# Opening of an FFT-mix-FFN kernel: padded x tiles, one tile of batch 1 ahead of the first step, and products of zeros on TensorE

## The chip, the core and the metric

The kernel runs on one NeuronCore of a Trainium2 chip. The metric is the device time in microseconds (us) from launch to end, the median of several executions. Engines are named as in the profile: PE (TensorE matmul), PEld (its weight load), DVE (VectorE), ACT (ScalarE), POOL (GpSimd), SP (SyncE, which here only issues DMAs). SPq and ACTq are DMA issues of SP and ACT.

## The reference

`x` is 2 batches of 3008 tokens by 256 values, all float32.

```python
X = np.fft.rfft(x, axis=1)
Yr = Xr @ w_r - Xi @ w_i + b_r          # Xr, Xi: parts of X
Yi = Xr @ w_i + Xi @ w_r + b_i
Yr, Yi = soft-threshold of each by 0.01
x = np.fft.irfft(Yr + 1j * Yi, n=3008, axis=1).reshape(6016, 256)
h = x @ w_in                            # 256 -> 2048, first layer
x = (np.maximum(h, 0) + alpha * np.minimum(h, 0)) @ w_out
h = x @ w_in2                           # second layer
y = (0 below -1, h above 1, (h + 1)**2 / 4 between) @ w_out2
```

## The kernel before

3008 = 47 * 64, so the transform over tokens is done in two stages. Stage A is a transform of length 47: `x` is laid out by the host as 16 tiles (`TILES`), 8 of each batch (`TILES_PER_BATCH`), each of 94 rows padded to 96 (`ROWS_PAD`) by 1024 columns. `real47(t, banks)` (L1058) multiplies one tile by the 96x96 constant `fwd_sb` in two products of 512 columns (two matmul records each). ACT copies the left half out of PSUM and DVE the right half, both called `copy_a`; ACT's `store_a` (L570) then stores the tile (384 KB) to the DRAM tensor `slots_scratch`. For tile 7, the last of batch 0, the left half is stored from ACT (L574) and the right half from SP (L355).

Stage B goes in 48 steps, two to a pair, 24 steps to a batch. A pair reads `zt` (256 KB, values of all 8 tiles of its batch, from `slots_scratch`) and `gc` (256 KB, constants of its two steps). Per step PE runs `forward` (2 products), `mix` of the step before (12 products with the split weights `wm_hi`, `wm_lo`) and `inverse` of the step before that (one product). ACT and DVE split and threshold between them, and `take_v` copies the result out for its store. So the first step of batch 0 needs all 8 tiles of batch 0 stored, but none of batch 1; the first step of batch 1 (step 24) needs tiles 8 to 15.

`FIRST_TILES` = 11: tiles 0 to 10 go through stage A ahead of step 0. Tiles 11 to 15 are `LATE_TILES`: each goes between `forward` and `mix` of step 1, 4, 7, 10 or 13. SP issues the loads in an order written out by hand (L342 to L365): the left half of x tile 0, `fwd_sb`, its right half, x tiles 1 to 8, `wm_raw` (512 KB), `gc` of pair 0, x tile 9, the bias; then it waits for the products of tile 6 and issues x tile 10; then it waits for the right half of tile 7 and stores it; then it waits until all nine stores of batch 0 have landed (L357) and issues `zt` of pair 0, x tile 11, `zt` and `gc` of pairs 1 and 2, x tile 12. From pair 3 on (loop at L367) each turn issues `zt` (when the forward products that read the slot before are done) and `gc`, in turns 4, 5 and 7 also the late x tile of `LATE_LOADS`, and then waits for a pair of `take_v` before it stores that pair.

`wm_hi` is made by ACT after tile 8 (L584 to L586), `wm_lo` by DVE after tile 9 (L816 to L819); PE waits for `wm_lo` in step 0 (L1208).

After step 47 come the two layers, in blocks of products with split operands (L1123), which the change doesn't touch. Their PSUM banks and SBUF areas are shared with stages A and B; `x_sb` and `a_sb` lie where the weights and token tiles of the layers stand later.

## Time and profile before

| | us |
|---|---|
| median of 3 runs | 1200.5 |
| lowest, highest | 1198.73, 1201.2 |
| the profiled execution | 1200.99 |
| its span, first to last instruction | 1198.9 |
| PE busy in the span | 1174.6 (98%) |
| DVE, ACT, POOL busy | 883.2, 850.3, 682.9 |

Stage A and the wait for step 0 take the first 32 us, the steps until about 170 us, and the two layers the rest. All that the change touches lies ahead of step 14, some 75 us from the start. "Granted clock" is the share of TensorE's full clock that the chip gave it: 1.00 is 2.4 GHz and 0.50 is 1.2 GHz.

### The profile page before, as it was taken

The page shows a single profiled execution, that of the slowest core. Times are in us where ns is not written, and L with a number is a line of the kernel's source. Part 1 is how long each engine was busy: PE and PEld are TensorE (multiplying, and loading weights), DVE is VectorE, ACT ScalarE, POOL GpSimd, SP SyncE. Part 2 cuts the span into 40 slices and gives each one's busy share as a digit, 9 for nine tenths or more (in the row PEclk, how much of TensorE's full clock was granted, in tenths as well). Part 3 has the DMA queues.
Part 4 walks back from the last instruction along what each step waited for, and adds up shares of the span by engine and source line. Part 5 has one row for each costly group of instructions (what it writes and reads, how often), then busy time and mean ns, then how long its engine had stood idle before and what let it go on. Part 6 is the DMA issues. An engine that isn't in the chain of part 4 may idle for free.

```text
span 1198.9 us, 21022 instructions
## 1 busy us (share of the span) xinstructions
PE 1174.6 (98%) x6944; PEld 1135.9 (95%) x6944; DVE 883.2 (74%) x1681; ACT 850.3 (71%) x1874; POOL 682.9 (57%) x714
## 2 busy tenths in 40 slices
PE   7899999999999999999999999999999999999997
PEld 2699889999999999999999999999999999999997
DVE  2577777777777777777778777877778787878765
ACT  2235556767776777767677788888878787878775
POOL 0005635666675757757556656565657565757553
PEclk9899999999999999999999999999999999999999
DMA  9777720211102111112004510101010101000001
GB/s 307 213 223 242 226 71 2 84 43 60 41 27 84 49 54 41 53 58 75 18 2 157 181 51 1 27 1 27 1 27 1 27 1 22 7 17 11 12 16 27
DMA packets 63772, 77.46 MB, mean 65 GB/s; under 512 B 30960, under 2 KB 43376, under 8 KB 63664
## 3 DMA queue, kind: packets, MB, share of 16 engines
q1 hardware_dynamic: 60180, 69.65, 19.3%
q10 hardware_dynamic: 3484, 6.48, 1.6%
q8 instruction: 55, 0.90, 0.3%
q14 instruction: 53, 0.43, 0.1%
HBM read 45.83 MB, written 30.28 MB: 63 GB/s over the span
## 4 chain that ended last, share of the span: by engine, by line
PE 93%; POOL 3%; DMA 1%; ACT 1%; DVE 1%; issue 1%; POOLq 0%; SPq 0%; DVEq 0%; ACTq 0%
PE bank L1123 79%; PE bank L1090 6%; PE bank L1109 2%; PE bank L1066 2%; PE bank L1100 2%; PE bank L1077 2%; POOL g_lo L498 2%; DMA slots_scratch<-a_sb 1%; DMA x_sb<-x 0%; POOL prep_raw L524 0%; POOL xc_lo L473 0%; ACT g_hi L745 0%; DMA fwd_sb<-fwd 0%; ACT prep_hi L768 0%; DVE y_sum L837 0%
## 5 line engine op out<-in xcount | busy, mean ns | idle before, releaser
L498 POOL TENSOR_TENSOR g_lo<-g_sb,g_hi 128x376 fp32r<-128x376 f32 x510 | 505.2, 1001 | 374.0 <-ACT g_hi L745 373.6
L1123 PE MATMUL bank<-g_hi,w_out_hi 128*128 128x376 f32 x1024 | 344.9, 337 | 0.9 <-POOL g_lo L498 0.4
L1123 PE MATMUL bank<-g_lo,w_out_hi 128*128 128x376 f32 x1024 | 342.0, 334 | 0.0
L1123 PE MATMUL bank<-g_hi,w_out_lo 128*128 128x376 f32 x1024 | 341.8, 334 | 0.0
L1123 PE MATMUL bank<-xc_hi,w_in_hi 128*128 128x376 f32 x896 | 302.3, 337 | 0.6 <-DVE partial L902 0.2
L1123 PE MATMUL bank<-xc_hi,w_in_lo 128*128 128x376 f32 x896 | 300.3, 335 | 0.0
L1123 PE MATMUL bank<-xc_lo,w_in_hi 128*128 128x376 f32 x896 | 298.5, 333 | 0.0
L745 ACT ACTIVATE g_hi<-g_sb 128x376 fp32r<-128x376 f32 x512 | 261.0, 510 | 44.2 <-DVE g_sb L939 28.5
L1123 PEld LDWEIGHTS bank<-g_hi,w_out_hi 128*128 128x128 f32 x1024 | 192.4, 188 | 8.8 <-POOL g_lo L498 7.6
L1123 PEld LDWEIGHTS bank<-g_lo,w_out_hi 128*128 128x128 f32 x1024 | 192.3, 188 | 0.0
L1123 PEld LDWEIGHTS bank<-g_hi,w_out_lo 128*128 128x128 f32 x1024 | 192.3, 188 | 0.0
L1123 PEld LDWEIGHTS bank<-xc_hi,w_in_hi 128*128 128x128 f32 x896 | 168.3, 188 | 1.6 <-DVE partial L902 0.5
L1123 PEld LDWEIGHTS bank<-xc_hi,w_in_lo 128*128 128x128 f32 x896 | 168.3, 188 | 0.1
L1123 PEld LDWEIGHTS bank<-xc_lo,w_in_hi 128*128 128x128 f32 x896 | 168.3, 188 | 0.0
L734 ACT ACTIVATE act_a<-bank,half 128x376 f32<-128x376 f32 x192 | 108.8, 566 | 45.6 <-PE bank L1123 44.7
L736 ACT ACTIVATE act_a<-act_a 128x376 f32<-128x376 f32 x256 | 132.9, 519 | 8.1
L939 DVE SCALAR_TENSOR_TENSOR g_sb<-bank,neg_alpha,g_sb 128x376 f32<-128x376 f32 x192 | 115.7, 602 | 2.5 <-ACT bank L730 2.3
L729 ACT ACTIVATE g_sb<-bank 128x376 f32<-128x376 f32 x192 | 91.8, 478 | 35.1 <-PE bank L1123 33.9
L912 DVE TENSOR_TENSOR partial<-u,bank 128x376 f32<-128x376 f32 x128 | 69.4, 542 | 62.8 <-PE bank L1123 61.9
L943 DVE SCALAR_TENSOR_TENSOR g_sb<-bank,act_a 128x376 f32<-128x376 f32 x192 | 104.4, 544 | 5.3 <-ACT act_a L736 1.2
L919 DVE TENSOR_TENSOR h<-partial,bank 128x376 f32<-128x376 f32 x128 | 69.7, 545 | 46.5 <-PE bank L1123 46.4
L730 ACT ACTIVATE bank<-bank 128x376 f32<-128x376 f32 x192 | 92.1, 480 | 0.0
(77 smaller groups left out, 1525.9 us busy)
## 6 DMA issues: line engine op xcount, KB each, us to landing
gc<-group_consts SPq DMA_DIRECT2D x24, 256.0 KB, 4.3
zt<-slots_scratch SPq DMA_DIRECT2D x24, 256.0 KB, 4.2
inverse_scratch<-v_sb SPq DMA_DIRECT2D x24, 256.0 KB, 2.5
ut<-inverse_scratch SPq DMA_DIRECT2D x16, 384.0 KB, 5.1
x_sb<-x SPq DMA_DIRECT2D x15, 384.0 KB, 8.1
slots_scratch<-a_sb ACTq DMA_DIRECT2D x15, 384.0 KB, 6.2
prep_raw<-wpack SPq DMA_DIRECT2D x16, 256.0 KB, 2.6
out<-yt SPq DMA_DIRECT2D x120, 32.0 KB, 1.6
```

Source lines behind the costliest of these rows:

```text
L498: pool.tensor_tensor(g_lo[kind][:, :], g_sb[n % 3][:, :], g_hi[kind][:, :].bitcast(f32), ALU.subtract)\
L729: act.activation(gg, h, ACT.Relu)
L730: act.activation(h, h, ACT.Relu, scale=-1.0).then_inc(act_done, 1)
L734: act.activation(a, h, ACT.Relu, bias=half[:, 0:1], scale=0.5).then_inc(root_ready, 1)
L736: act.activation(a, a, ACT.Square).then_inc(act_done, 1)
L745: act.activation(g_hi[kind][:, :], g_sb[n % 3][:, :], ACT.Copy).then_inc(hi_ready, 1)
L912: dve.tensor_tensor(partial[:, :], u2[:, :], c21_bank[:, 0:N], ALU.add).then_inc(u3_ready, 1)
L919: dve.tensor_tensor(h22[:, :], partial[:, :], c12_bank[:, 0:N], ALU.add).then_inc(h_ready[C22], 1)
L939: dve.scalar_tensor_tensor(out=gg, in0=h_of(kind), scalar=neg_alpha[:, f:f + 1], in1=gg, op0=ALU.mult, op1=ALU.add).then_inc(g_ready, 1)
L943: dve.scalar_tensor_tensor(out=gg, in0=h_of(kind), scalar=1.0, in1=a, op0=ALU.max, op1=ALU.min).then_inc(g_ready, 1)
L1090: last = pe.matmul(y_bank[:, 0:D], xs[s % SLOTS][:, c, at:at + P], ws[:, (part * DC + c) * D:(part * DC + c + 1) * D], start=n == 0, stop= ...
L1123: done = pe.matmul(out_ap, w, g, start=first and n == 0, stop=last_one and n == 2, skip_group_check=unchecked)
```

## The change

- The host pads each x tile to 128 rows (512 KB instead of 384 KB), `x_sb` gets 128 partitions and `fwd_sb` 128 rows with zeros below row 96. Each tile but the first is one transfer as before. The products now contract over 128 rows. `a_sb` and the stores stay at 96 rows.
- `FIRST_TILES` is 9: only tile 8 of batch 1 goes ahead of step 0. Tiles 9 to 15 go into steps 1, 3, 5, 7, 9, 11 and 13. SP loads x tile 9 after `zt` of pair 0, x tile 10 where x tile 12 stood, and x tiles 11 to 15 in turns 3 to 7 of its loop.
- SP stores the right half of tile 7 ahead of `gc` of pair 0 and `wm_raw`, which stood ahead of it, and the bias goes behind x tile 9. The wait for the products of tile 6 is gone.
- `wm_hi` and `wm_lo` are made after the copies of all nine first tiles, and PE waits for `wm_lo` ahead of the first `mix` instead of in step 0.
- PE runs 2 products of zeros (96x96 by 96x512, `WARM_PRODUCTS`) before it waits for `fwd_sb`, and 3 more (`WAIT_PRODUCTS`) after tile 8, ahead of step 0. They write `xt_bank[0]`, which step 0 overwrites. DVE clears the operand first, ahead of its other clears.

```diff
-FIRST_TILES = TILES_PER_BATCH + 3
-LATE_TILES = {1: FIRST_TILES, 4: FIRST_TILES + 1, 7: FIRST_TILES + 2, 10: FIRST_TILES + 3, 13: FIRST_TILES + 4}
-LATE_LOADS = {4: FIRST_TILES + 2, 5: FIRST_TILES + 3, 7: FIRST_TILES + 4}
+FIRST_TILES = TILES_PER_BATCH + 1
+LATE_TILES = {1 + 2 * n: FIRST_TILES + n for n in range(TILES - FIRST_TILES)}
+LATE_LOADS = {3 + n: FIRST_TILES + 2 + n for n in range(TILES - FIRST_TILES - 2)}
+WARM_PRODUCTS = 2
+WAIT_PRODUCTS = 3
...
-        x_sb = sb("x_sb", [ROWS_PAD, TILES, TILE_COLS], scope=step_a)
+        x_sb = sb("x_sb", [P, TILES, TILE_COLS], scope=step_a)
...
-        fwd_sb = sb("fwd_sb", [ROWS_PAD, ROWS_PAD], scope=fft)
+        fwd_sb = sb("fwd_sb", [P, ROWS_PAD], scope=fft)
...
-            for t in range(1, TILES_PER_BATCH + 1):
+            for t in range(1, FIRST_TILES):
                 load_x(t)
-            sp.dma_start(wm_raw[:, :], wmix).then_inc(wm_in, 16)
-            load_matrices(0)
-            load_x(TILES_PER_BATCH + 1)
-            sp.dma_start(bias_sb[:, :], bias).then_inc(bias_in, 16)
-            sp.wait_ge(a_done, 2 * (TILES_PER_BATCH - 1))
-            load_x(TILES_PER_BATCH + 2)
             t = TILES_PER_BATCH - 1
             sp.wait_ge(a_right, t + 1)
             sp.dma_start(az_rows[0, 0:ROWS_PAD, t * TILE_COLS + HALF_COLS:(t + 1) * TILE_COLS],
                          a_tile(t)[:, HALF_COLS:]).then_inc(a_stored[0], 16)
+            load_matrices(0)
+            sp.dma_start(wm_raw[:, :], wmix).then_inc(wm_in, 16)
             sp.wait_ge(a_stored[0], 16 * (TILES_PER_BATCH + 1))
             load_values(0)
             load_x(FIRST_TILES)
+            sp.dma_start(bias_sb[:, :], bias).then_inc(bias_in, 16)
...
-                if t == TILES_PER_BATCH:
-                    act.wait_ge(wm_in, 16)
-                    act.activation(wm_hi[:, :], wm_raw[:, :], ACT.Copy).then_inc(wm_hi_ready, 1)
+            act.wait_ge(wm_in, 16)
+            act.activation(wm_hi[:, :], wm_raw[:, :], ACT.Copy).then_inc(wm_hi_ready, 1)
...
+            dve.memset(a_tile(TILES - 1)[:, 0:HALF_COLS], 0.0).then_inc(idle_ready, 1)
             dve.memset(half[:, :], 0.5).then_inc(half_ready, 1)
...
-                if t == TILES_PER_BATCH + 1:
-                    dve.wait_ge(wm_hi_ready, 1)
-                    dve.tensor_tensor(wm_lo[:, :], wm_raw[:, :], wm_hi[:, :].bitcast(f32), ALU.subtract)\
-                       .then_inc(wm_lo_ready, 1)
+            dve.wait_ge(wm_hi_ready, 1)
+            dve.tensor_tensor(wm_lo[:, :], wm_raw[:, :], wm_hi[:, :].bitcast(f32), ALU.subtract)\
+               .then_inc(wm_lo_ready, 1)
...
+            def idle_products(count):
+
+                zeros = a_tile(TILES - 1)
+                for _ in range(count):
+                    pe.matmul(xt_bank[0][0:ROWS_PAD, :], zeros[:, 0:ROWS_PAD], zeros[:, 0:HALF_COLS],
+                              start=True, stop=True)
+
+            pe.wait_ge(idle_ready, 1)
+            idle_products(WARM_PRODUCTS)
             pe.wait_ge(fwd_in, 16)
...
             def mix(s):
+                if s == 0:
+                    pe.wait_ge(wm_lo_ready, 1)
                 pe.wait_ge(xt_lo_ready, s + 1)
...
                 real47(t, [a_bank[(2 * t + part) % 4] for part in range(2)])
+            idle_products(WAIT_PRODUCTS)
             for s in range(STEPS):
                 forward(s)
                 if s in LATE_TILES:
                     real47(LATE_TILES[s], a_bank[0:2])
-                if s == 0:
-                    pe.wait_ge(wm_lo_ready, 1)
-                else:
+                if s:
                     mix(s - 1)
...
-    tiles = np.zeros((TILES, ROWS_PAD, TILE_COLS), x.dtype)
+    tiles = np.zeros((TILES, P, TILE_COLS), x.dtype)
```

## Rows read from the trace of the kernel before

**Rows 1.** The page, parts 1 and 2: busy time, and the clock in 40 slices.
```profile
PE 1174.6 (98%) x6944; PEld 1135.9 (95%) x6944; DVE 883.2 (74%) x1681; ACT 850.3 (71%) x1874; POOL 682.9 (57%) x714
...
PEclk9899999999999999999999999999999999999999
```

**Rows 2.** The chain that ended last, first 60 us: start us, us, what.
```profile
3.32 17.22 PE bank L1066 x32
...
21.27 7.56 DMA slots_scratch<-a_sb
...
28.85 0.39 SPq L322
...
29.28 5.66 DMA x_sb<-x
...
46.47 1.72 PE bank L1066 x4
48.19 1.42 PE bank L1090 x12
49.61 0.43 PE bank L1100 x2
50.05 0.44 PE bank L1077 x4
```

**Rows 3.** PE in order of time: start us, us, line, records [idle before, releaser].
```profile
24.92 1.96 PE L1066 MATMUL bank<-x_sb,fwd_sb 96*96 96x512 f32 x4 [2.69 <-DMA x_sb<-x]
27.65 1.96 PE L1066 MATMUL bank<-x_sb,fwd_sb 96*96 96x512 f32 x4 [0.77 <-DVE a_sb L812]
32.23 1.16 PE L1077 MATMUL bank<-gc,zt 128*128 128x128 f32 x8 [2.63 <-DMA zt<-slots_scratch]
34.98 3.73 PE L1066 MATMUL bank<-x_sb,fwd_sb 96*96 96x512 f32 x4 [1.59 <-DMA x_sb<-x]
```

**Rows 4.** Weight loads of two records and a copy, in order of time.
```profile
9.40 0.28 PEld L1066 LDWEIGHTS bank<-x_sb,fwd_sb 96*96 96x96 f32 x1 [0.57 <-issue]
...
10.49 0.16 PEld L1066 LDWEIGHTS bank<-x_sb,fwd_sb 96*96 96x96 f32 x1 [0.27 <-issue]
...
22.27 0.69 DVE L812 COPY a_sb<-bank 96x512 f32<-96x512 f32 x1 [1.03 <-PE bank L1066]
```

**Rows 5.** Stretches: us, busy PE, PEld, DVE, ACT, POOL, clock, DMA share, GB/s.
```profile
8.00:11.00 3.00, 3.00 (x6) 0.97 (x5) 0.69 (x1) 0.59 (x1) 0.00 (x0) 1.00 1.01 244
14.00:17.00 3.00, 3.00 (x9) 1.14 (x8) 1.06 (x2) 1.05 (x2) 0.00 (x0) 1.00 1.03 416
...
50.00:80.00 30.00, 30.00 (x210) 26.32 (x209) 22.65 (x59) 12.06 (x36) 0.00 (x0) 1.00 0.70 214
...
34.00:35.00 1.00, 0.02 (x1) 0.02 (x1) 0.72 (x3) 0.00 (x0) 0.00 (x0) 0.50 0.95 349
...
40.00:41.00 1.00, 1.00 (x8) 1.00 (x8) 0.00 (x0) 0.00 (x0) 0.00 (x0) 0.71 1.06 265
```

**Rows 6.** The tile wm_raw: ns min/median/max, first and last start us; its load's landing.
```profile
L347 SPq DMA_DIRECT2D wm_raw<-wmix x1: 671/671/671, 6.2 to 6.2; - x1
L586 ACT ACTIVATE wm_hi<-wm_raw x1: 1056/1056/1056, 23.4 to 23.4; 128x1024 fp32r<-128x1024 f32 x1
L818 DVE TENSOR_TENSOR wm_lo<-wm_raw,wm_hi x1: 1211/1211/1211, 27.5 to 27.5; 128x1024 fp32r<-128x1024 f32 x1
...
DMA to landing us min/median/max: 14.8/14.8/14.8
```

**Rows 7.** A store issue of ACT, in order of time.
```profile
30.41 0.31 ACTq L578 DMA_DIRECT2D slots_scratch<-a_sb  x1
```

**Rows 8.** DMA issues from 45 to 80 us: count, KB each, median us to landing.
```profile
inverse_scratch<-v_sb SPq DMA_DIRECT2D x6, 256.0 KB, 2.5
...
slots_scratch<-a_sb ACTq DMA_DIRECT2D x4, 384.0 KB, 3.6
x_sb<-x SPq DMA_DIRECT2D x3, 384.0 KB, 5.0
```

More of the change, by code:

```diff
@@ L206, in fft_mix_ffn_kernel @@
         rims_ready = sem("rims_ready")
+        idle_ready = sem("idle_ready")
         wm_hi_ready = sem("wm_hi_ready")
@@ L1267 @@
     fwd47, inv, group_consts = transform_constants()
+    fwd = np.zeros((P, ROWS_PAD), fwd47.dtype)
+    fwd[:ROWS_PAD] = fwd47
     rows_bias = np.concatenate([np.broadcast_to(v, (N2, D)) for v in (b_r, b_i)], axis=0)
@@ L1274 @@
         "wpack": np.stack(layers),
-        "fwd47": fwd47,
+        "fwd47": fwd,
         "inv47": inv,
```

## The prediction

> **What bounds the kernel now.** I read the page first: PE is busy 98% of the span, and the clock row shows less than full speed only in the second slice, 30 to 60 us [rows 1]. So time can be won only where PE stands still or runs at half clock, and every piece of PE work that is added outside such a place costs its full length. The chain of waits says where the first 60 us go [rows 2]: tiles 0 to 7 on PE from 3.32 to 20.54; the store of the last half tile, issued at 21.27, takes 7.56 us and lands at 28.83; then zt of pair 0 and x tile 11, the latter issued at 29.28 and landed at 34.94. From 34.98 on the chain is PE alone. PE in order of time [rows 3] shows the same from its side: tiles 9 and 10 fall into the wait for the store and cost nothing; PE idles 2.63 us before the two forward products at 32.23 and 1.59 us before tile 11 at 34.98. That tile takes 3.73 us [rows 3], the one at 46.47 takes 1.72 [rows 2].
>
> The clock: the granted clock is 0.50 (1.2 GHz) at 34 us, after PE had been busy for only 1.16 of the 5.4 us from 29.6 to 34.98, and back at 1.00 during 40 to 41 us [rows 3, 5], 5.4 us after tile 11 began. At the start the profile's clock column shows 1.00, but the weight loads of the tiles take 0.28 us with 0.57 idle ahead of them, 0.85 us a record, at 9.40, and 0.16 with 0.27, 0.43 us a record, at 10.49 [rows 4]: PE there runs at half speed until about 9.8, 6.5 us after its first product. A product is two records, 1.7 us at half clock and 0.86 at full.
>
> DMA: from 8 to 11 us only x loads move, at 244 GB/s with all 16 engines busy; from 14 to 17 loads and stores together move 416 GB/s [rows 5]. wm_raw was issued at 6.2 and landed 14.8 us later [rows 6], so SP's queue was full of loads when the last store was put behind them.
>
> **The change part by part.** The sum is made against the profiled execution, 1200.99 us, of which the span is 1198.9; it lies 0.5 us above the median of the runs shown, and I take the difference as carried over.
>
> 1. Warm products. The clear of 96x512 on DVE isn't in the trace; the copy of the same shape from PSUM is 0.69 us [rows 4], so it is between 0 and 0.7, and PE starts at about 1.3. Two products at half clock take 2 x 1.72 = 3.4 us, to 4.75. The first real product, which started at 3.32, starts at 4.75: a loss of 1.4. The clock then comes up 5.4 to 6.5 us after 1.3, at 6.7 to 7.9, instead of at 9.8. Tiles 0 to 7 hold 16 products of 0.86 us at full clock, 13.8 us, plus half of the time spent at half clock: 4.75 + 13.8 + (7.3 - 4.75)/2 = 19.8, against 20.54 now (20.4 by the same formula). Gain 0.7; bounds: a gain of 1.0 with the clock up at 6.7, and a loss of 1.4 if it comes up only 6.5 us after the first real product, as now.
>
> 2. Padding. At 244 GB/s a tile of 384 KB (0.393 MB) takes 1.6 us. What 512 KB in 128 rows takes alone isn't in the trace. From below: at the 416 GB/s that the engines reach in the later stretch, 1.26 us. From above: at 244 GB/s, 2.15 us. I take about 1.5, since the engines show that they can move 416 while the 96-row loads alone get 244; what holds those is then not the engines but the spread of the rows. Then x tile 8 is in by 16 us, PE never waits for a tile, and padding is worth nothing in itself. In the words of the Trainium skill (SBUF — State Buffer, Door 1: The DMA port swizzle), rows 0 to 63 reach only half of the SBUF's ports and rows 64 to 127 the other half; a 96-row tile would then be limited by the 64 rows on the first half and cost as much as one of 128. The low rate of the 96-row loads agrees; that 128 rows are better no row here shows.
>
> 3. The last store. SP's issues ahead of it drop from 16 to 11: wm_raw, gc, the bias and x tiles 9 and 10, 1.7 MB, no longer stand before it, against 1.2 MB of padding. The queues hold the stores alone once the x loads are in. Nine x tiles are 4.7 MB; at 1.5 us each they end near 16. About 1.2 MB of stores wait by then, PE makes 223 GB/s of them (0.393 MB in 1.72 us), and the engines move up to 416, so little is left at 20.5. The half tile is issued at 20.6 and lands between 22.9 (2.3, just under the 2.5 of 256 KB stores [rows 8]) and 24.2 (3.6, a 384 KB store there). I take 23.3, against 28.83 [rows 2]: gain 5.5.
>
> 4. zt of pair 0. Issued at 28.85 it landed at 32.2, 3.4 us later [rows 2, 3], with next to nothing queued in front. Now gc and wm_raw (0.79 MB), issued right after the store, are partly ahead of it, and the store of tile 8 beside it: 0.3 to 0.6 us more. It lands at 27.0; bounds 26.2 and 28. Two forward products follow as now.
>
> 5. x tile 9, issued behind zt. Tile 11 landed 2.7 us after zt, with a store of 384 KB (tile 10's) beside it [rows 7]. Now no store is beside it, but 512 KB are to move: 1.5 to 2.7, I take 2.0. PE starts the late tile of step 1 at 29.0 instead of 34.98: 6.0 earlier.
>
> 6. wm_lo. wm_raw lands at about 25.5; ACT's split and DVE's take 1.06 and 1.21 us [rows 6], so wm_lo is there by 28, ahead of the first mix at 30.7 at the earliest. ACT's wait for wm_raw holds back its first split_xt, which isn't due before 27.6; DVE's wait for wm_hi holds back nothing else. Nothing, as long as wm_raw is not a further 2.7 us late.
>
> 7. Two more late tiles. Tiles 9 and 10 leave a wait in which they were free and enter steps in which PE is busy all of the time (30.00 of 30 us from 50 to 80 [rows 5]). Each adds 1.72 us [rows 2]: a loss of 3.44, with no doubt about it. A step without a tile is 1.43 + 0.43 + 0.44 = 2.30 us.
>
> 8. Wait products. Three at full clock are 2.6 us, from the end of tile 8 (21.5) to 24.1, ahead of zt's landing: they cost nothing unless zt comes before 24.1. What they are worth is the clock at 29. Without them PE would idle from 21.5 to 27; with them it idles 24.1 to 27.0, works 1.16, idles about 0.9. That is 1.16 us of work in 4.9, hardly more than the 1.16 in 5.4 that let the clock fall now, and less than the 1.96 us in 5.4 from 22.2 to 27.65 that did not [rows 3]. So I take it that the clock falls again, and 5.4 us at half clock, 2.7 us lost, stay as they are. Bounds: 0 and a gain of 2.7.
>
> 9. Late loads. zt, gc, a pair's store, a tile's store and x (512 KB) are 1.70 MB in two steps of 6.33 us, 269 GB/s, where 50 to 80 us now show 214 at a share of 0.70: a share of up to 0.88 by bytes. An x tile is issued some 1.9 us after the end of a step with a tile and is needed 9.1 us after that end, so it has 7.2 us; the loads now take 5.0 [rows 8]. It fits; nothing. A load above 7.2 us would not (rival D).
>
> Sum: 6.0 - 3.44 = 2.5 us gained, and items 1, 3 and 4 are in the 6.0. All later work is behind PE and moves up with it. 1200.5 - 2.5 = 1198.0.
>
> **The rivals.** A, the forecast: the clock falls again, 1198.0, own range 1196.8 to 1199.3 by items 3 to 5. Chance 0.42.
>
> B: the clock stays up over the shorter gap, since zt comes by 26.5 or since a gap of 2.7 us, like the one at 24.92, leaves it [rows 3]. Then 2.7 more is won, less about 0.5: tile 9 starts at 29.0, step 3 needs x tile 10 at 34.9, and some 1.9 MB are in front of it. 1200.5 - 2.5 - 2.2 = 1195.8; with zt 1 us earlier 1194.8. In its favour: PE's work before the gap ends later relative to zt than now. Against: the gap and the work in it look like those at 30 to 35. The Trainium skill (TensorE: Matmul & The Clock Gate, Why this matters for your kernels) says that the clock only drops after a sufficiently long gap between bursts, which would make this the outcome; the drop at 34 us came over two gaps of 2.63 and 1.59 with work between. Chance 0.30.
>
> C: padding costs its bytes, 2.15 us a tile at 244 GB/s. Loads alone until 13 us, then half of 416 beside stores: x tile 7 lands near 20.5, PE ends it at 22.3, the store lands at 25.3, zt at 28.9, x tile 9 at 31.1. That is 3.9 earlier than now, less 3.44: 0.5 gained, 1200.0. For it: rate is all that the row gives. Against: 416 GB/s on the same engines. Chance 0.12.
>
> D, the other side: x tiles 12 to 15 come late to their steps. The place is the wait in real47 of steps 7, 9, 11, 13; it decides once a load takes over 7.2 us instead of 5.0, which a DMA share near 1 would bring: 269 GB/s stand against 214/0.70 = 306 by [rows 5], and 128 rows need only cost somewhat more than their bytes. Each then costs 1 to 1.8 us; at 1.4, 5.6 us in all, 1198.0 + 5.6 = 1203.6. It passes no change at 0.6 us a tile and 0.2% slower at 1.25. Chance 0.10.
>
> E: the products of zeros don't bring the clock up sooner, 2.1 us worse in item 1, of which the time that the stores get to drain hides about 1: 1199.1. Chance 0.06.
>
> **How the numbers follow.** A difference of 0.2%, 2.4 us, is about what a measurement of this kernel can tell from none, so faster is below 1198.1 and slower above 1202.9. A lies at this edge: 0.42 x 0.55 = 0.23 to faster, 0.19 to the same; B 0.29 faster, 0.01 the same; C 0.11 the same, 0.01 slower; E 0.01 faster, 0.05 the same; D 0.02 the same, 0.08 slower. Faster 0.53, same 0.38, slower 0.09. The range goes from 1194.2 (B with an early zt) to 1201.0 (C with its bounds), which leaves out D and the ends.
>
> **What would show it.** Step 1: weight loads 0.43 us apart from about 7.5 us on. Step 2: over 300 GB/s between 4 and 11 us; 244 would be rival C. Step 3: the landing of SP's last store at about 23.3. Steps 4 and 5: forward products at 27.0, tile 9 at 29.0. Step 7: seven tiles at 1.72 us in the chain. Step 8: a granted clock of 0.50 somewhere between 27 and 34; 1.00 throughout is rival B. Step 9: no wait of PE for x_sb after 30 us; some in steps 7 to 13 are rival D. The prediction is wrong if the first mix is not 5 to 7 us earlier than now, or if later steps take longer than 2.30 and 4.02 us.

## The result, and the profile after

| | before | after |
|---|---|---|
| median, both kernels in turn on one chip | 1200.7 | 1202.8 |
| lowest, highest of 22 runs each | 1198.39, 1203.02 | 1200.64, 1207.63 |
| ratio, 95% interval | | 1.002 [1.0011, 1.0028] |
| the profiled execution, its span | 1200.99, 1198.9 | 1201.93, 1199.9 |

The change makes the kernel 2.1 us slower. The forecast was 2.5 us faster, and 1202.8 lies above the range.

The page of the changed kernel: the span, the busy time of each engine, and the clock row.

```profile
span 1199.9 us, 21044 instructions
PE 1179.9 (98%) x6954; PEld 1139.0 (95%) x6954; DVE 883.8 (74%) x1682; ACT 850.4 (71%) x1874; POOL 682.8 (57%) x714
...
PEclk9999999999999999999999999999999999999999
```

PE is busy 5.3 us longer than before. The five products of zeros alone are 6.4 us (3.7 for the first two, 2.7 for the last three, below); most of that lies in waits, but the first two put off the first real product, from 3.32 us [rows 2] to 4.96. The half-clock mark has left the second slice [rows 1], but that isn't all gain: the next views tell.

PE in order of time, the changed kernel (columns as in rows 3).

```profile
1.45 3.73 PE L1058 MATMUL bank<-a_sb 96*96 96x512 f32 x4 [1.45 <-DVE a_sb L803]
4.96 2.96 PE L1074 MATMUL bank<-x_sb,fwd_sb 128*96 128x512 f32 x4
8.18 10.54 PE L1074 MATMUL bank<-x_sb,fwd_sb 128*96 128x512 f32 x24 [0.26 <-DMA x_sb<-x]
18.88 1.96 PE L1074 MATMUL bank<-x_sb,fwd_sb 128*96 128x512 f32 x4 [0.16 <-DMA x_sb<-x]
21.25 1.96 PE L1074 MATMUL bank<-x_sb,fwd_sb 128*96 128x512 f32 x4 [0.41 <-DMA x_sb<-x]
23.04 2.74 PE L1058 MATMUL bank<-a_sb 96*96 96x512 f32 x6
29.38 2.08 PE L1085 MATMUL bank<-gc,zt 128*128 128x128 f32 x8 [3.60 <-DMA zt<-slots_scratch]
31.25 3.46 PE L1074 MATMUL bank<-x_sb,fwd_sb 128*96 128x512 f32 x4
```

The two warm products (1.45 to 4.96), nine tiles, the three wait products (to 25.8), then 3.60 us of nothing until `zt`, the forward products at 29.38 and tile 9 at 31.25. Before, the same points were 32.23 and 34.98 [rows 3]. Tile 9 thus starts 3.7 us earlier, where 6.0 were forecast.

SP's issues of the same stretch, and those that store pairs 2 and 7 of batch 0 (here and below "the third store" and "the eighth store").

```profile
21.59 0.34 SPq L352 DMA_DIRECT2D slots_scratch<-a_sb  x1
21.98 0.42 SPq L319 DMA_DIRECT2D gc<-group_consts  x1
22.45 0.48 SPq L355 DMA_DIRECT2D wm_raw<-wmix  x1
24.82 0.38 SPq L325 DMA_DIRECT2D zt<-slots_scratch  x1
25.24 1.21 SPq L314 DMA_DIRECT2D x_sb<-x  x1
...
55.97 0.38 SPq L329 DMA_DIRECT2D inverse_scratch<-v_sb  x1
...
84.18 0.38 SPq L329 DMA_DIRECT2D inverse_scratch<-v_sb  x1
```

The same two stores in the profile of before:

```profile
59.13 0.37 SPq L326 DMA_DIRECT2D inverse_scratch<-v_sb  x1
...
85.62 0.38 SPq L326 DMA_DIRECT2D inverse_scratch<-v_sb  x1
```

When the eighth store is issued all late tiles of either kernel are done, so its time is a ruler for everything that the change touches. The change was 3.16 us ahead at the third store, and 1.44 ahead at the eighth, with one late tile more in between (1.72). What is left of the span after the eighth store is 1113.3 us in the kernel before (1198.9 - 85.6) and 1115.7 in the changed one (1199.9 - 84.2), though nothing there was edited. So two questions: why is the lead at 85 us only 1.4, and where do 2.4 us go behind it?

### The profile page after: what moved, and what is told of

Same layout as the page of the kernel before. It is cut to its first block, busy times and chain, and to the rows that moved or that the text cites. A ratio compares the mean times of both kernels' runs of the same rounds, so it can differ in the third digit from the quotient of the medians.

```text
span 1199.9 us, 21044 instructions
## 1 busy us (share of the span) xinstructions
PE 1179.9 (98%) x6954; PEld 1139.0 (95%) x6954; DVE 883.8 (74%) x1682; ACT 850.4 (71%) x1874; POOL 682.8 (57%) x714
## 4 chain that ended last, share of the span: by engine, by line
PE 78%; POOL 3%; issue 1%; ACT 0%; DVE 0%; POOLq 0%; DVEq 0%; ACTq 0%
PE bank L1133 76%; PE bank L1119 2%; POOL g_lo L498 2%; POOL prep_raw L524 0%; POOL xc_lo L473 0%; POOL prep_raw L509 0%; ACT g_hi L744 0%; ACT prep_hi L767 0%; POOL prep_raw L514 0%; POOL prep_raw L512 0%; POOL prep_raw L510 0%; POOLq L138 0%; ACT bank L729 0%; DVE yt L965 0%; ACT act_a L733 0%
```

## Experiments

Times are medians; "before" is the kernel before, run in turn with the variant on the same chip. The experiments were run in four sets on three chips, and each set has its own "before"; across sets the ratios are the safer comparison. The interval of a ratio is 0.0008 to 0.0018 to either side, 1 to 2 us, so two variants are told apart only from some 2 us on; smaller differences rest on the profiles, and each of those is one execution. No kernel here leaves out a part of the computation: products of zeros and of `wm_raw` go to banks that are overwritten.

**The parts one by one.** No products of zeros:

```diff
-WARM_PRODUCTS = 2
-WAIT_PRODUCTS = 3
+WARM_PRODUCTS = 0
+WAIT_PRODUCTS = 0
```

> The changed kernel without products of zeros (0 instead of 2 and 3). The changed kernel's median is 2.1 us above before (ratio 1.002), though in its profile the steps run 1.44 us ahead of before up to step 34. Theory 1, the zeros pay: the half-clock stretch at the start lasts some 1.4 us longer for real products and the one ahead of step 0 comes back, so 1 to 3 us slower than the changed kernel, ratio to before 1.003 to 1.0045. Theory 2, the zeros cost (they push back the first product and bring nothing): ratio 1.000 to 1.001.

Measured 1203.79, before 1200.82: 1.002 [1.0007, 1.0033]. The last half tile was stored at 23.57 instead of 21.59, tile 9 began at 33.45 instead of 31.25, the eighth store went out at 86.76 instead of 84.18. In time 1.0 us is left of that by medians and nothing by ratios (1.002 for both), inside the noise: neither expectation is confirmed.

Unpadded, the rest of the change as it is (`fwd_sb` is back to 96 rows too):

```diff
-        x_sb = sb("x_sb", [P, TILES, TILE_COLS], scope=step_a)
+        x_sb = sb("x_sb", [ROWS_PAD, TILES, TILE_COLS], scope=step_a)
...
-    tiles = np.zeros((TILES, P, TILE_COLS), x.dtype)
+    tiles = np.zeros((TILES, ROWS_PAD, TILE_COLS), x.dtype)
```

> The changed kernel with x tiles of 96 rows as before; all else as changed. Theory 1, padding is neutral or helps (378 GB/s in the stretch 8 to 11 us of the changed kernel against 244 before): ratio to before 1.002 to 1.003. Theory 2, the padded bytes are what costs (x loads beside the stores, late tiles): ratio 1.000 or below, and the last store lands before 24.0 instead of 24.8.

Measured 1202.23, before 1200.82: 1.001 [0.9992, 1.0027]. SP's store and its `zt` in this kernel:

```profile
20.25 0.32 SPq L352 DMA_DIRECT2D slots_scratch<-a_sb  x1
...
23.58 0.38 SPq L325 DMA_DIRECT2D zt<-slots_scratch  x1
```

Both are issued 1.3 us earlier than with 128 rows (21.59, 24.82). Most of that lead is gone at tile 9 (30.99 against 31.25), since `zt` took 5.5 us here, and the time is the same within the noise.

The reverse, the kernel before with padding alone:

> The kernel before with x tiles padded to 128 rows and nothing else. Theory 1: TensorE sets the pace of tiles 0 to 7 anyway, so the ratio is 0.9995 to 1.0005. Theory 2, the added bytes stand ahead of the last store: it lands later than 28.83 by 1 to 3 us, ratio 1.001 to 1.0025.

Measured 1201.73, before 1200.82: 1.0004 [0.999, 1.0019]. Its weight loads show the price, first this kernel and then the kernel before:

```profile
8.73 0.39 PEld L1066 LDWEIGHTS bank<-x_sb,fwd_sb 128*96 128x96 f32 x2 [2.79 <-DMA x_sb<-x]
```

```profile
5.99 0.28 PEld L1066 LDWEIGHTS bank<-x_sb,fwd_sb 96*96 96x96 f32 x1 [0.57 <-DMA x_sb<-x]
```

x tile 1 is used at 8.73 instead of 5.99, PE stands, and the last half tile is stored at 23.58 instead of 21.27. In this profile padding is not neutral in stage A. The wait for the store doesn't hide it: the store landed at 31.4 instead of 28.8 and `zt` at 34.4 instead of 32.2, as the second expectation had it. But the clock was back earlier after tile 11, the eighth store went out only 0.7 us later (86.33), and in time nothing is told apart.

**Is it the long wait?** A real tile in place of two products of zeros, x tile 9 loaded right behind the store, and `wm_raw` behind `zt`:

```diff
-FIRST_TILES = TILES_PER_BATCH + 1
+FIRST_TILES = TILES_PER_BATCH + 2
-WAIT_PRODUCTS = 3
+WAIT_PRODUCTS = 1
...
+            load_x(TILES_PER_BATCH + 1)
             load_matrices(0)
-            sp.dma_start(wm_raw[:, :], wmix).then_inc(wm_in, 16)
             sp.wait_ge(a_stored[0], 16 * (TILES_PER_BATCH + 1))
             load_values(0)
+            sp.dma_start(wm_raw[:, :], wmix).then_inc(wm_in, 16)
```

> The changed kernel, but tile 9 (the second of batch 1) goes ahead of step 0 too, with one product of zeros behind it instead of three; its x load stands right behind the last store and wm_raw behind zt of pair 0. Six late tiles instead of seven. Theory 1, each late tile costs 1.72 us of TensorE and the wait for zt has room for it: 1.7 us below the changed kernel or more, ratio to before 1.000 to 1.001. Theory 2, what costs is not the late tiles: ratio 1.002 as the changed kernel. A zt that lands over 1.7 us later because of the x load ahead of it would also give 1.002.

Measured 1201.27, before 1200.82: 1.0004 [0.999, 1.0018]. Eighth store at 84.00, against 84.18 in the change. The real tile found no free time: its load landed at 28.1, PE stood 5.2 us for it and ran it at half clock, and `zt`, which had landed at 30.4, was first read at 33.2. By its interval the time is told apart neither from before nor from the change.

**The late tiles alone.** The kernel before with 9 first tiles and seven late ones, every load where it was (`wm_lo` is made after the copy of tile 8, the last of the first tiles, instead of tile 9):

```diff
-FIRST_TILES = TILES_PER_BATCH + 3
-LATE_TILES = {1: FIRST_TILES, 4: FIRST_TILES + 1, 7: FIRST_TILES + 2, 10: FIRST_TILES + 3, 13: FIRST_TILES + 4}
+FIRST_TILES = TILES_PER_BATCH + 1
+LATE_TILES = {1 + 2 * n: FIRST_TILES + n for n in range(TILES - FIRST_TILES)}
...
```

> The kernel before with the late tiles of the change alone: tiles 9 and 10 go into steps 1 and 3, the others into 5 to 13, their loads and all other DMAs stay where they are, no padding, no zeros. Theory 1, a late tile costs its 1.72 us of TensorE and its place ahead of step 0 was free: 3.4 us slower than before, ratio 1.0025 to 1.003; more if the longer idle stretch ahead of step 0 keeps the clock down longer. Theory 2, the steps hide part of it: ratio below 1.0015.

Measured 1203.44, before 1201.4: 1.0015 [1.0002, 1.0029]. It costs about as much as the whole change. `zt` landed at 30.0, against 32.2 in the profile of before: with two tiles fewer the queues are emptier.

**A clock fall outside the change.** At about 148 us the first token products wait 2.43 us for DVE in both kernels. Granted clock and busy times of PE from 140 to 160 us (columns as in rows 5), before and then after:

```profile
140.00:160.00 20.00, 16.71 (x131) 15.90 (x130) 14.34 (x38) 10.46 (x30) 11.54 (x13) 1.00 0.30 93
```

```profile
140.00:160.00 20.00, 16.72 (x118) 15.86 (x117) 12.88 (x34) 9.07 (x26) 10.47 (x11) 0.91 0.30 93
```

In the changed kernel the clock fell there, in the one before it did not. To take this away from both, five products are put into step 42, in the stretch ahead of the wait:

```diff
+                if s == 42:
+                    for _ in range(5):
+                        pe.matmul(xt_bank[(s + 1) % SLOTS][:, 0:D], wm_raw[:, 0:P], wm_raw[:, 0:D],
+                                  start=True, stop=True)
```

On the kernel before:

> The kernel before with five products (128x128 by 128x256, read from wm_raw, into a PSUM bank that is free then) in step 42, in the 2.43 us in which TensorE waits near 148 us for DVE. All up to 145 us is as before, so its profile is a second look at the front of the kernel before. Theory 1: the clock falls at that gap in some executions (it did in the profile of the changed kernel, 140 to 160 us at 0.91, 1.5 us lost, and not in that of before), so the fill gives 0.3 to 1.5 us, ratio 0.999 to 0.9997. Theory 2: the fall has nothing to do with the gap, ratio 1.000 or, if the fill ends after the wait, 1.0003. For the front: if the profile shown of before was a typical execution, tile 11 starts at 35.0 and the third pair's store at 59.1; if it was a slow one, 1 us or more earlier.

Measured 1199.91, before 1201.4: 0.9987 [0.9974, 0.9999]. On the changed kernel:

> The changed kernel with the same five products in step 42. Theory 1, the clock at 150 us is what takes back the gain of the front: ratio to before 1.0005 or less and 1.5 us below the changed kernel. Theory 2, it is a matter of chance in both kernels alike: 0.3 to 0.8 us below the changed kernel, ratio 1.001 to 1.0018. A second look at the front of the changed kernel too: third pair's store at 55.97 if that profile was typical, later if it was a fast one.

Measured 1200.86, before 1201.4: 1.0000 [0.9989, 1.0010], where the change without it has 1.0020. It takes 1.5 us off the one, run in turn with it, and about 2 off the other (1.9 by medians, 2.4 by ratios, of two sets). In the nine profiles without these products the clock fell in five (the change, e1, e2, e3, e9) and not in four (before, e4, e5, e10); with them it never fell. e3 is the kernel before but for its rows, so the fall isn't the change's doing. Whether it comes more often in the changed schedule (four profiles of six) than in the one before (one of three) so few can't tell; the mean clocks below say no.

**More wait products.**

```diff
-WAIT_PRODUCTS = 3
+WAIT_PRODUCTS = 7
```

> The changed kernel with 7 products of zeros ahead of step 0 instead of 3. They end 3.4 us later, at about 29.1 by the changed kernel's profile, where the forward products start at 29.38 at half clock. Theory 1: the clock stays at 1.00, the forward products take 1.16 instead of 2.08 us and tile 9 1.7 instead of 3.5; 1.5 to 2.5 us below the changed kernel, ratio to before 1.0000 to 1.0007. Theory 2: zt often lands before 29 and the zeros hold it up, or the clock is not what the front waits for: ratio 1.0015 to 1.002.

Measured 1201.55 (11 runs), before 1201.4: 0.9997 [0.9984, 1.0011], against 1.0020 for the change. The execution that was profiled took 2340 us and is left out, so no profile shows what the seven products did to the clock.

**The order of the queue.** The change with `gc` and `wm_raw` ahead of the store again:

```diff
+            load_matrices(0)
+            sp.dma_start(wm_raw[:, :], wmix).then_inc(wm_in, 16)
             t = TILES_PER_BATCH - 1
             sp.wait_ge(a_right, t + 1)
...
-            load_matrices(0)
-            sp.dma_start(wm_raw[:, :], wmix).then_inc(wm_in, 16)
```

> The changed kernel with one part undone: gc of pair 0 and wm_raw are issued right behind x tile 8 again, ahead of the last store. Theory 1 (what the change moved ahead of the store it put ahead of zt, so it won next to nothing): the store lands 1 to 2 us later than 24.8, but zt 3.3 us after its issue instead of 4.5, so zt lands at 29.3 to 30.0 against 29.3 and the time is that of the changed kernel within 0.6 us, ratio to before 1.001 to 1.002. Theory 2 (the prediction's: issuing the store first is worth most of the 5.5 us): zt lands at 31 or later, 2 us above the changed kernel or more, ratio 1.003 or more.

Measured 1202.01, before 1201.17: 1.0004 [0.9996, 1.0013]. Its store, its `zt`, and PE's wait for it:

```profile
20.43 0.34 SPq L354 DMA_DIRECT2D slots_scratch<-a_sb  x1
...
26.04 0.38 SPq L325 DMA_DIRECT2D zt<-slots_scratch  x1
```

```profile
28.81 2.08 PE L1085 MATMUL bank<-gc,zt 128*128 128x128 f32 x8 [4.48 <-DMA zt<-slots_scratch]
```

The store lands 5.6 us after its issue instead of 3.2, `zt` 2.7 instead of 4.5. The forward products start at 28.81, against 29.38 in the change, and the time is no longer: storing first wins nothing.

`gc` ahead of the store, and `wm_raw` behind `zt` and x tile 9:

> The changed kernel with gc of pair 0 issued behind x tile 8 (256 KB ahead of the last store) and wm_raw behind x tile 9 (nothing between the last store and zt). Theory 1: zt lands 3.3 us after its issue instead of 4.5, near 28.3, x tile 9 near 29.6 instead of 30.6; 0.7 to 1.3 us below the changed kernel, ratio to before 1.0003 to 1.001. Theory 2: the 4.5 us of zt come from the store of tile 8 beside it or from the read of fresh data, not from wm_raw: zt lands 4.3 us or more after its issue, ratio 1.0015. wm_lo gets ready by about 32.5; if the first mix waits for it, the gain is gone by that.

Measured 1204.37, before 1201.17: 1.0025 [1.0013, 1.0036], the worst. PE and its weight loads:

```profile
27.48 1.16 PE L1085 MATMUL bank<-gc,zt 128*128 128x128 f32 x8 [2.61 <-DMA zt<-slots_scratch]
```

```profile
35.38 0.29 PEld L1100 LDWEIGHTS bank<-wm_hi,xt_hi 128*128 128x128 f32 x1 [3.61 <-DVE wm_lo L817]
```

`zt` lands 1.9 us earlier (27.4) and its forward products still run at full clock, but the first mix now waits for `wm_lo`. The tile view of `wm_raw` shows why:

```profile
L358 SPq DMA_DIRECT2D wm_raw<-wmix x1: 432/432/432, 25.8 to 25.8; - x1
L585 ACT ACTIVATE wm_hi<-wm_raw x1: 1056/1056/1056, 32.4 to 32.4; 128x1024 fp32r<-128x1024 f32 x1
L817 DVE TENSOR_TENSOR wm_lo<-wm_raw,wm_hi x1: 1224/1224/1224, 33.5 to 33.5; 128x1024 fp32r<-128x1024 f32 x1
...
DMA to landing us min/median/max: 6.6/6.6/6.6
```

Issued at 25.8 it lands at 32.4, and the two splits (1.06 and 1.22) end at 34.7.

**Two lines of improvement.** The changed kernel with 96 rows, the order of e10, six wait products and the fill of step 42:

> The changed kernel with all that the runs speak for: x tiles of 96 rows, wm_raw behind x tile 9 as in the run before, 6 products of zeros ahead of step 0, and the five products in step 42. By the parts (each against the changed kernel: rows 0.7, order 1.0, zeros 2.0, step 42 2.2, less overlap) 4 to 5 us below the changed kernel, 1198 to 1199, ratio 0.998 to 0.999. If the late tiles are what costs, it stays 1 us or more above the next run all the same.

Measured 1201.5, before 1201.17: 0.9998 [0.9988, 1.0008], 3 us short of what the parts promised. The six zeros did hold the clock over `zt`: the forward products ran at full clock from 27.65 and tile 9 took 1.96 us. Then the mix waited for `wm_lo`, as in e10, and the clock fell in that wait:

```profile
34.18 0.29 PEld L1100 LDWEIGHTS bank<-wm_hi,xt_hi 128*128 128x128 f32 x1 [4.09 <-DVE wm_lo L817]
```

So the late load that e10 had shown to be a fault was in this kernel too, and e11 doesn't say what the changed schedule can reach. The kernel before with two warm products, two products of zeros after tile 8, three after tile 10, and the fill:

```diff
...
             for t in range(FIRST_TILES):
                 real47(t, [a_bank[(2 * t + part) % 4] for part in range(2)])
+                if t == TILES_PER_BATCH:
+                    idle_products(2)
+            idle_products(WAIT_PRODUCTS)
...
```

> The kernel before with 2 products of zeros at the start, 2 behind tile 8, 3 behind tile 10, and the five products in step 42; tiles, loads and order as before. Theory 1: the two late tiles of the change (3.4 us) cost more than its front wins, and the zeros (1 us at the start, up to 2.7 ahead of step 0) work on the old schedule as well: 2 to 3 us below before with step 42 alone, 1197 to 1198.5, ratio 0.9965 to 0.9985, below the run before this. Theory 2: the zeros hold up tile 9 or the forward products: no better than with step 42 alone, 0.9987.

Measured 1199.05 (8 runs), before 1201.17: 0.9979 [0.9965, 0.9993]. PE in order of time:

```profile
31.01 3.51 PE L1063 MATMUL bank<-a_sb 96*96 96x512 f32 x6
34.36 1.05 PE L1090 MATMUL bank<-gc,zt 128*128 128x128 f32 x8
```

The last three zeros ran at half clock, from 31.0, and ended after `zt` had landed at 32.76: they held up the forward products by 1.6 us. But it wasn't they that lost the clock: it had fallen at 25.7, during tile 9. Hence the last experiment but one, below.

**The late tiles again, with the fill.**

> The kernel before with the late tiles of the change alone (as in the run of late tiles alone), and with the five products in step 42, which take the fall of the clock at 148 us out of the comparison. Against before with step 42 alone (mean 1199.9). Theory 1: 3.4 us of TensorE less what an emptier DMA queue wins at the front (the store landed at 27.3 instead of 28.3 to 28.9 with late tiles alone, zt at 30.0 instead of 31.9 or 32.2): 1.0 to 2.0 us slower, 1201 to 1202. Theory 2, the full price: 1203.3.

Measured 1201.96 (11 runs), before 1200.25: 1.0011 [1.0001, 1.0022]. Against e6, the same without the two added late tiles, 0.9987: 0.0024 more, 2.9 us; by the means of the two (1201.76, 1199.85) 1.9 us. PE's wait for `zt`:

```profile
29.98 2.07 PE L1076 MATMUL bank<-gc,zt 128*128 128x128 f32 x8 [7.50 <-DMA zt<-slots_scratch]
```

With nothing changed but the tiles, `zt` lands at 29.9, as in e5, where before, e6 and e16, with the old schedule, have 31.8 to 32.4.

The reverse, the changed kernel with the fill, 11 first tiles and five late ones, x tiles 9 and 10 loaded behind tile 8:

```diff
-FIRST_TILES = TILES_PER_BATCH + 1
-LATE_TILES = {1 + 2 * n: FIRST_TILES + n for n in range(TILES - FIRST_TILES)}
-LATE_LOADS = {3 + n: FIRST_TILES + 2 + n for n in range(TILES - FIRST_TILES - 2)}
+FIRST_TILES = TILES_PER_BATCH + 3
+LATE_TILES = {1 + 3 * n: FIRST_TILES + n for n in range(TILES - FIRST_TILES)}
+LATE_LOADS = {4: FIRST_TILES + 2, 5: FIRST_TILES + 3, 7: FIRST_TILES + 4}
...
```

> The changed kernel with step 42 filled and with the late tiles undone: tiles 9 and 10 ahead of step 0 again, their loads behind x tile 8 as before; padding, the store ahead of gc and wm_raw, and the zeros (3 behind tile 10) stay. Against the changed kernel with step 42 filled (mean 1200.8). Theory 1: 3.4 us less in the steps, but 1 MB more is loaded and 0.8 MB more stored ahead of zt, so zt lands at about 32; 1 to 2 us faster, 1199 to 1200, ratio 0.998 to 0.999. Theory 2, the tiles in the steps are free by the early front: 1201 or slower.

Measured 1200.32, before 1200.25: 0.9995 [0.9983, 1.0007], 0.5 us below e7 of another set, inside the noise. SP's store and its `zt`:

```profile
20.30 0.34 SPq L354 DMA_DIRECT2D slots_scratch<-a_sb  x1
...
27.28 0.38 SPq L325 DMA_DIRECT2D zt<-slots_scratch  x1
```

Two tiles are out of the steps (3.4 us of PE), but their loads and a store are back in the queue, and the store takes 7.0 us instead of 3.2. Eighth store at 83.06, against 84.59 in e7: 1.5 of the 3.4 arrive.

**The best line.** e12 with one product of zeros after tile 10 instead of three:

> The run with zeros on the old schedule, with 1 product of zeros instead of 3 behind tile 10. There the three ran at half clock from 31.0 to 34.4, and zt had landed at 32.8, so they held up the forward products by 1.6 us. If they hold up more than they win in clock: 0.5 to 1 us faster than with 3, 1198.0 to 1198.6. If the clock pays for them: the same or slower, 1199.0 to 1200.

Measured 1197.67, before 1200.25: 0.9984 [0.9976, 0.9993]. It beats both kernels. By ratios it is not told apart from e12 (0.9979), nor from the fill of step 42 alone (e6, 0.9987), so no time shows that one product is better than three here. PE in order of time and the window from 30 to 40 us:

```profile
28.52 1.02 PE L1063 MATMUL bank<-a_sb 96*96 96x512 f32 x2
31.33 1.16 PE L1090 MATMUL bank<-gc,zt 128*128 128x128 f32 x8 [1.79 <-DMA zt<-slots_scratch]
32.36 1.96 PE L1079 MATMUL bank<-x_sb,fwd_sb 96*96 96x512 f32 x4
```

```profile
30.00:40.00 10.00, 8.64 (x57) 7.26 (x58) 5.44 (x15) 3.08 (x10) 0.00 (x0) 1.00 1.02 302
```

The clock is 1.00 throughout, the forward products take 1.16 us and tile 11 takes 1.96 instead of 3.73 [rows 3]. Up to the end of tile 10 this kernel is e12, whose clock had fallen at 25.7. What differs first between the two profiles is thus the execution and not the number of products.

**How much does one profile tell?** e6 once more, for one more profile of a front (all up to the eighth store) that is the kernel before's:

> The kernel before with step 42 filled, one more execution with a profile: a third look at the front of the kernel before. In the profile of before, the third pair's store is at 59.1, in the first run with step 42 filled at 56.2. Around 56 to 57 says that the profile shown was a slow front; 59 that it was usual.

One execution, 1200.04. The third and the eighth store of e6 and of e16:

```profile
56.17 0.37 SPq L326 DMA_DIRECT2D inverse_scratch<-v_sb  x1
...
82.66 0.38 SPq L326 DMA_DIRECT2D inverse_scratch<-v_sb  x1
```

```profile
57.80 0.37 SPq L326 DMA_DIRECT2D inverse_scratch<-v_sb  x1
...
84.29 0.38 SPq L326 DMA_DIRECT2D inverse_scratch<-v_sb  x1
```

The front of one and the same code ends at 82.66, 84.29 and, in the profile of before, 85.62: 3 us apart, mean 84.2. The eighth store of e7, a second profile of the changed front:

```profile
84.59 0.38 SPq L329 DMA_DIRECT2D inverse_scratch<-v_sb  x1
```

84.59, with 84.18 in the change itself: mean 84.4. On this count the front of the changed kernel is no earlier than that of the kernel before.

**The clock over all executions.** Beside its time every execution has its mean granted clock, rounded to 0.001. Means over each variant's executions, with those of "before" in the same set:

| | mean granted clock | before in its set | ratio of times |
|---|---|---|---|
| the change | 0.9941 | | 1.0020 |
| e1, no zeros | 0.9931 | 0.9938 | 1.0020 |
| e8, seven wait products | 0.9966 | 0.9941 | 0.9997 |
| e7, the change with the fill | 0.9962 | 0.9941 | 1.0000 |
| e6, before with the fill | 0.9957 | 0.9941 | 0.9987 |
| e5, late tiles alone | 0.9929 | 0.9941 | 1.0015 |
| e13, late tiles with the fill | 0.9945 | 0.9941 | 1.0011 |
| e15, before with zeros and fill | 0.9974 | 0.9941 | 0.9984 |

Since PE is busy 98% of the span, 0.001 of the clock is worth about 1.2 us (an estimate: 0.001 of 1200). The change has the clock of the kernel before (0.9937 to 0.9941 in the four sets), so its 2.1 us are not lost to the clock. The fill raises it in both, by about what it wins in time, and so do e8's seven products, which is the nearest to a profile of them that there is. Moving the late tiles alone lowers it by 0.0012 (e5 against its before, e13 against e6), some 1.4 us of the 2 to 3 that it costs. PE's idle stretch ahead of step 0 is 7.5 us and more in both; that this is what lowers it is likely and not shown.

## Why the prediction was wrong

**Item 1, warm products: right.** With 96 rows and the two zeros the last half tile is stored at 20.1 to 20.4 (e2, e11, e12, e15), without them at 20.3 to 21.5 (before, e5, e6, e13, e16): 0.65 us between the means, where 0.7 was forecast. Without them and with 128 rows (e1) it goes 2.0 us later than in the change, part of which is the late x tile 1 of item 2.

**Item 2, padding neutral: wrong, by up to 1.3 us.** The rate was right, and better than forecast. The window of the changed kernel from 8 to 11 us shows 385 GB/s (not the 378 of e2's expectation), 1.36 us a tile, against 244 [rows 5]; the other profiles have 365 to 419 with 128 rows and 250 to 279 with 96.

```profile
8.00:11.00 3.00, 2.82 (x7) 1.23 (x8) 1.34 (x2) 0.59 (x1) 0.00 (x0) 1.00 1.03 385
```

The step that failed is "PE never waits for a tile". PE's weight loads in the changed kernel:

```profile
8.18 0.24 PEld L1074 LDWEIGHTS bank<-x_sb,fwd_sb 128*96 128x96 f32 x2 [1.22 <-DMA x_sb<-x]
```

x tile 1 landed at 8.1, 2.2 us later than in the kernel before, since a good rate says nothing about when the first of many queued tiles is complete. There are shorter waits for x tiles 7 and 8 too. It cost 1.3 us at the last half tile (21.59 against 20.25 in e2). But it isn't a fixed price: with 128 rows x tile 1 landed anywhere from 6.7 to 8.7 us, with 96 from 5.8 to 7.1, and in e9 and e14, both padded, the last half tile was stored at 20.43 and 20.30. It wasn't rival C: the rate wasn't the limit. The window agrees in direction with the Trainium skill (SBUF — State Buffer, Door 1: The DMA port swizzle), by which the DMA rate depends on how many of the SBUF's ports the rows reach. That is not the prediction's "cost as much": a tile of 128 rows moved in less time than one of 96 (1.36 us against 1.6).

**Items 3 and 4, the store and `zt`: the step that failed, with item 7.** The store took 3.2 us from its issue at 21.6 and landed at 24.8: 4.0 earlier than before, not 5.5, and beyond item 3's bounds (22.9 and 24.2). One us of the miss is item 2's late issue. But `zt`, issued behind `gc` and `wm_raw`, took 4.5 us, where I had allowed 3.4 and 0.3 to 0.6 more. The lines L325 and L352:

```profile
L325 SPq DMA_DIRECT2D zt<-slots_scratch x1: 378/378/378, 24.8 to 24.8; - x1
...
DMA to landing us min/median/max: 4.5/4.5/4.5
```

```profile
L352 SPq DMA_DIRECT2D slots_scratch<-a_sb x1: 345/345/345, 21.6 to 21.6; - x1
...
DMA to landing us min/median/max: 3.2/3.2/3.2
```

It landed at 29.3, not at 27.0, and outside the bounds of item 4 (26.2 and 28): with that the 6.0 us of the sum became 3.7. e9 and e10 give the reason: the DMA engines are busy (336 to 363 GB/s between 27 and 29 us), and the store, `gc`, `zt`, `wm_raw` and x tile 9 are all needed by 35. With 0.79 MB behind the store, `zt` is late; with it ahead, the store is; with `wm_raw` last, `wm_lo` is. I had counted what stands ahead of the store, and not what then stands ahead of `zt`. (Item 3's 223 GB/s for PE's stores is 229, 0.393 MB in 1.72 us; nothing hangs on it.)

**Item 5: the number right by luck.** Tile 9 began 1.9 us after `zt` landed (2.0 forecast). Its load was in earlier, 1.3 us after `zt`, below the bounds of 1.5 and 2.7; what held PE were the forward products at half clock (2.08 instead of 1.16). All of it was 2.25 later than forecast.

**Item 6: right, with the margin nearly used up.** `wm_raw` landed at 27.7 instead of 25.5, and up to 2.7 us more was allowed. The split cost nothing in the change, and PE waited 3.6 us for it in e10, where the load landed at 32.4.

**Item 7, two late tiles for 3.44: right for PE's time, and counted apart from what it is tied to.** In the steps each costs 1.7: the lead falls from 3.16 to 1.44 between the third and the eighth store. But taking the two tiles out of the wait also takes a store and loads of 0.8 MB from in front of the last store and `zt`. That alone brings `zt` 2.2 us forward (e5 and e13: 30.0 and 29.9 us, against a mean of 32.1 of the three profiles with the old schedule), and the whole change, with its new order of issues, brings it 2.6 (29.3, and 29.7 in e7). So some 0.4 us is left for all the rest, the order of the issues included, on which item 3 had built. Moved alone the tiles cost 1.8 to 2.9 us (e5, e13), and moved back alone they bring about 0.5 in time and 1.5 at the eighth store (e14). "With no doubt" was true of PE's time and not of the path; the gain of items 3 to 5 was mostly this same move, and moving the tiles also lowered the clock, which no term had.

**Item 8, the clock falls again: right.** Windows of the changed kernel behind the wait products, which ended at 25.8:

```profile
27.00:28.00 1.00, 0.00 (x0) 0.00 (x0) 0.00 (x0) 0.28 (x1) 0.00 (x0) 0.80 1.10 363
28.00:29.00 1.00, 0.00 (x0) 0.00 (x0) 0.18 (x1) 0.78 (x1) 0.00 (x0) 0.50 1.00 336
34.00:35.00 1.00, 1.00 (x6) 0.60 (x5) 0.25 (x1) 0.00 (x0) 0.00 (x0) 0.78 1.06 343
```

It fell to 0.50 (1.2 GHz) within 27 to 28 us, some 2 us after the three zero products had ended, in one wait of 3.60 us, and came back during 34 to 35, 5 us after the forward products had begun. Before it came back at 40 to 41 [rows 5], so half-clock time moved with the wait rather than going away. In e7, the same code, it fell only at 30.1. The row that item 8 leaned on, work of 1.96 us up to 27.65 "that did not" let it fall, was chance too: in e6 and e16, the same code up to there, it fell at 25.5 and 24.9. Rival B was wrong for three products. With six (e11) the clock held over `zt` and tile 9, and e8 has rival B's gain in time and in its mean clock. e15's window shows what it looks like on the old schedule.

**Item 9: right.** PE waits for no x tile from 31.25 on.

**The sum.** At tile 9 the change is 3.7 ahead, not 6.0, and two tiles take 3.4 of it. That would leave 0.3 at the eighth store, and 1.44 is left: the clock was back some 3 us after the start of tile 9, where it had needed 5.6 after that of tile 11. At half clock half of the time is lost, so the difference is worth 1.2 us. Forecast were 2.5. The profile of before that the sum was made against had the latest of three fronts; against their mean the lead at the eighth store is nothing. So 1.1 of the missing 2.5 is the mis-sized sum, and 1.4 is the profile that it was set against: one execution whose front lies that far from the mean of three, although the three runs alone already span 2.5 us. That leaves the change equal at the eighth store; that it ends slower is not in the sum at all.

**Outside the forecast.** Behind the eighth store the changed kernel's profile is 2.4 us longer. 2.0 of it lies behind the wait at 148 us: from its end to the last instruction it is 1050.6 us, against 1048.6. Over the nine profiles without the fill this stretch is 1050.2 to 1050.8 where the clock fell and 1048.6 to 1049.1 where it didn't, so the fall is its cause. 0.3 is a wait for `ut` at the first token products, which reads what the steps stored. With the fill, 1113.7 (e6, e16) stand against 1115.1 (e7): the clock no longer falls, and 1.04 of that 1.4 is the wait for `ut`.

```profile
130.58 1.10 PE L1119 MATMUL bank<-inv_sb,ut 96*128 96x94 f32 x8 [1.04 <-DMA ut<-inverse_scratch]
```

It stands in most profiles of the changed schedule (0.3 to 1.4 us; none in e1), and in e13, e14 and e15 (0.65, 0.4, 0.85), but not in those of before, e3, e5, e6 or e12, and hardly in e16 (0.2). So it isn't bound to the change.

**What stands, and how firmly.** Shown by its time: the change is slower, by 2.1 us by medians (1.3 to 3.4 by the interval of the ratio); late tiles moved alone cost about 2 (0.2 to 3.5 by the interval of e5); the fill of step 42 gains 1.5 to 2.4. Seven wait products gain 1.3 by medians and 2.8 by ratios, at the edge of what can be told. Shown by profiles: the reordering that only moves the wait, and the three zeros that don't hold the clock; padding's late first tile in most of them. Worked out and not shown: e7 is 0.95 us slower than e6 by medians (1.6 by ratios), for which the fronts (84.4 against 84.2) and the wait for `ut` (about 1) would do. e5's profiled execution is the fastest of its twelve and e13's nearly so, so their eighth stores (85.33, 84.34) don't locate what the late tiles cost. How the whole of 2.1 is shared out isn't settled, since every share is near the width of the intervals; that it isn't the clock the mean clocks say. Open too: why the first load of `ut` takes 5.5 to 6.6 us instead of 5.0 to 5.4 in some kernels, and why the first 128-row tile often lands late while the rate is higher.

## What to carry to other kernels

Where the DMA engines are full until the first step can start, changing the order of the transfers only chooses which needed one lands last: list all that must be in by then and ask what the move puts in front of the next. Work that fills a wait is free only there; taking it out is paid in full elsewhere, unless its own transfers were what made the wait long, and then both effects are one term. Cheap filler products that end close to the end of the wait keep the clock up where ones that end early don't (six in the one profile of e11, seven by e8's time and clock, against three), and they turn into a delay when they run on past it, the more so at half clock (e12). Before a sum of 2 us is set against one profile, compare the same stretch in a second profile of the same code; and when times differ by no more than that, compare the mean granted clocks of all executions before giving the clock the blame or the credit.

## What the runs showed of the hardware

- From 8 to 11 us, where only loads move, 365 to 419 GB/s were moved with x tiles of 128 rows (385 in the change), against 244 to 279 with 96. Yet the first whole tile, x tile 1, landed at 6.7 to 8.7 us with 128 rows and at 5.8 to 7.1 with 96.
- The same code doesn't get the same clock. After the three zero products, which end at 25.8 and 25.9, it fell between 27 and 28 us in the change and at 30.1 in e7; in the kernel before it fell at 33.7, in e6 at 25.5 and in e16 at 24.9. Over a single wait of 2.43 us at 148 us it fell in five of nine executions, which cost 1.8 us between the means.
- Products of zeros and of unneeded data count as work: with two of them ahead of the first tile full speed came at about 5 to 8.5 us (ten profiles), without at 8 to 13 (seven), and with five in step 42 the fall at 148 us never came (eight profiles).
- A 256 KB load (the first `zt`) took 2.7 to 4.2 us from issue to landing where SP had issued nothing just ahead of it (2.7 in e9), and 4.5 to 5.5 with 0.79 MB just issued (the change, e1, e2, e7). A 192 KB store took 2.7 to 3.3 us with the loads issued behind it (3.2 in the change), and 5.4 to 8.4 with `wm_raw` or x tiles 9 and 10 ahead of it (5.6 in e9, 7.0 in e14).
- Executions of the same code ended their first 85 us up to 3 us apart, and all 131 executions of the kernel before that ran beside the experiments have a median of 1200.82 with a standard deviation of 1.93.
